# The first matmul of each MLP layer by Strassen's seven block products

## The chip, the cores and the metric

The kernel runs on one core of a Trainium2 chip. The metric is the device time of one execution in microseconds: 992.04 us is the median of 3 runs before the change (991.65 to 992.12).

## The reference

Causal attention with a decay over 4 x 8 heads of 576 tokens and width 64 is followed by two MLP layers over all 2304 tokens. Everything is float32.

```
scores = q @ k.T / 8 + decay, causal;  attn = softmax(scores) @ v      # (2304, 512) over all heads
h = x @ w_in            # 512 -> 2048
g = relu(h) ** 2        # layer 1
x = g @ w_out           # 2048 -> 512
h = x @ w_in            # layer 2
g = h where h >= 1, 0 where h <= -1, else (h + 1) ** 2 / 4
out = g @ w_out
```

## The kernel before

Each float32 operand of a matmul is split into a high part (rounded to the type fp32r) and a low part (the rest), and each product is three matmuls: high x high, high x low, low x high. The high part is a copy on ScalarE, the low part a subtraction on VectorE (on GpSimd for q, k, v and the first weights).

The attention goes over 16 pairs of heads as a software pipeline. The order of the work on each engine is written out by hand in lists (PE_ORDER, ACT_ORDER, DVE_ORDER, and PE_LAST, ACT_LAST, DVE_LAST for the last step, in which the first pieces of layer 1 stand among the last ones of the attention). The letters are pieces of work: T transposes of probabilities and their splits, O products with v, R the reciprocals of the sums, M the writing of x, U the first matmul of a tile, W a weight split, G a g tile.

The MLP layers then take the tokens in five chunks of 384, 512, 512, 512 and 384. In a chunk, j runs over the 16 tiles of 128 columns of the hidden width. `up(layer, c, j)` (L1140 to L1168) computes h of tile j from 4 slices of the model width, 12 matmuls, into one of four PSUM banks. ScalarE and VectorE turn h into g, high and low (`relu2`, L702 and L908, in layer 1; `smooth2`, L712 and L915, in layer 2). `down1` (L1172) and `down2` (L1189) add tile j's part of the second matmul into four other banks, 12 matmuls in a chunk of 512; in layer 1 g streams and w_out is stationary, in layer 2 it is the other way round. TensorE runs up of tile j ahead of down of tile j - 2.

All weights of a layer lie in SBUF, high and low (W). They are loaded once a layer through the sync queue (`load_w`, L434) and split once. GpSimd splits the first four weight tiles and the first x chunk during the last attention steps and then has nothing more to do. At the end of a chunk ScalarE and VectorE copy y from PSUM to x (`put_y1`, `put_y2`); the last chunk is stored tile by tile (L498 to L504).

All engines are in order and wait for each other by counting semaphores.

## Time and profile before

| | us |
|---|---|
| median of 3 runs | 992.04 |
| profiled execution | 991.63 |
| its span on the core | 989.80 |
| TensorE (PE) busy | 983.0 |
| VectorE (DVE) busy | 516.8 |
| ScalarE (ACT) busy | 405.3 |
| GpSimd (POOL) busy | 153.0 |

The profiler records each instruction of one execution. The page has busy times and the clock over 40 slices of the span; other views are tables by stretch of time, groups of instructions by source line and shape, the chain of waits, and the instructions in order of time. Times of single instructions are us from the span's start. Matmuls are pipelined: their own durations overlap, so their pace is read from the starts of successive groups.

### The profile page before, as it was taken

The numbers are of one execution on the slowest core, as the hardware profiler recorded it, in microseconds if no ns is written. First come the engines' busy times: TensorE is split into PE (matmuls) and PEld (weight loads), VectorE is DVE, ScalarE is ACT, GpSimd is POOL, SyncE is SP. The second block draws the span as 40 slices with busy tenths as digits, with TensorE's granted clock in tenths as the row PEclk, the third lists the DMA queues.
The fourth block names the chain that finished last, engine by engine and source line by source line (L and its number), as shares of the span: only waits on it lengthen the run. The fifth ranks groups of instructions, "written<-read, shape, count | busy, mean of one in ns | idle before, by whom it ended". The sixth has DMA issues, their size and how long they took to land.

```text
span 989.8 us, 14986 instructions
## 1 busy us (share of the span) xinstructions
PE 983.0 (99%) x5266; PEld 859.0 (87%) x5266; DVE 516.8 (52%) x1079; ACT 405.3 (41%) x888; POOL 153.0 (15%) x208
## 2 busy tenths in 40 slices
PE   8999999999999999999999999999999999999998
PEld 7888888999988888888889998988888888888997
DVE  7888888765422332232233566555455445544544
ACT  7888888854322232232223454232222223223322
POOL 7877888600000000000000000000000000000000
PEclk9999999999999999999999999999999999999999
DMA  6445555232000000000002440000001000000100
GB/s 220 147 145 177 158 175 195 65 121 72 1 1 1 1 0 0 0 0 1 1 1 64 127 129 22 1 32 1 1 1 43 0 0 33 10 1 1 43 1 32
DMA packets 39473, 50.01 MB, mean 51 GB/s; under 512 B 2656, under 2 KB 26720, under 8 KB 39424
## 3 DMA queue, kind: packets, MB, share of 16 engines
q1 hardware_dynamic: 39424, 49.37, 15.6%
q8 instruction: 30, 0.49, 0.2%
q14 instruction: 19, 0.16, 0.1%
HBM read 44.56 MB, written 4.79 MB: 50 GB/s over the span
## 4 chain that ended last, share of the span: by engine, by line
PE 96%; DVE 2%; ACT 1%; issue 0%; DMA 0%
PE banks L1167 39%; PE banks L1198 19%; PE banks L1184 19%; PE banks L1121 7%; PE banks L1066 5%; PE banks L1076 5%; PE banks L1092 1%; PE banks L1125 1%; PE banks L1117 0%; ACT W L689 0%; DMA fs<-f_dram 0%; DVE W L894 0%; DVE r L928 0%; DVE r L922 0%; ACT r L716 0%
## 5 line engine op out<-in xcount | busy, mean ns | idle before, releaser
L1167 PE MATMUL banks<-xs,W 128*128 128x512 f32 (+1 forms) x1728 | 383.7, 371 | 0.0
L1167 PEld LDWEIGHTS banks<-xs,W 128*128 128x128 f32 x1728 | 317.9, 188 | 47.4
L1198 PE MATMUL banks<-W,gs 128*128 128x512 f32 x864 | 209.1, 390 | 0.2 <-DVE gs L905 0.2
L1184 PE MATMUL banks<-gs,W 128*128 128x512 f32 (+1 forms) x960 | 209.0, 367 | 0.0
L1184 PEld LDWEIGHTS banks<-gs,W 128*128 128x128 f32 x960 | 175.1, 188 | 22.5
L1198 PEld LDWEIGHTS banks<-W,gs 128*128 128x128 f32 x864 | 161.7, 188 | 32.9 <-DVE gs L905 0.5
L905 DVE TENSOR_TENSOR gs<-r,gs 128x512 fp32r<-128x512 f32 (+1 forms) x160 | 102.3, 639 | 113.0 <-ACT gs L710 62.1
L716 ACT ACTIVATE r<-r 128x512 f32<-128x512 f32 (+1 forms) x80 | 47.2, 590 | 217.2 <-DVE r L924 217.2
L912 DVE TENSOR_TENSOR r<-r 128x512 f32<-128x512 f32 (+1 forms) x80 | 51.0, 638 | 160.9 <-ACT r L707 160.9
L707 ACT ACTIVATE r<-banks 128x512 f32<-128x512 f32 (+1 forms) x80 | 44.3, 554 | 177.3 <-PE banks L1167 176.5
L922 DVE TENSOR_SCALAR r<-banks 128x512 f32<-128x512 f32 (+1 forms) x80 | 50.9, 636 | 76.0 <-PE banks L1167 75.7
L1121 PE MATMUL banks<-pT,vs 128*128 128x448 f32 (+2 forms) x384 | 86.9, 348 | 0.0
L660 ACT ACTIVATE pr<-pr,nmax 128x576 f32<-128x576 f32 (+2 forms) x144 | 82.7, 581 | 0.6 <-DVE nmax L862 0.6
L928 DVE TENSOR_TENSOR r<-banks,r 128x512 f32<-128x512 f32 (+1 forms) x80 | 51.1, 639 | 50.2 <-ACT r L716 50.0
L710 ACT ACTIVATE gs<-r 128x512 fp32r<-128x512 f32 (+1 forms) x80 | 47.2, 590 | 70.3 <-DVE r L912 53.8
L847 DVE TENSOR_TENSOR pT<-banks,pT 128x256 fp32r<-128x256 f32 (+1 forms) x144 | 70.0, 515 | 7.7 <-ACT pT L666 5.9
L666 ACT ACTIVATE pT<-banks 128x256 fp32r<-128x256 f32 (+1 forms) x144 | 61.5, 459 | 25.7 <-PE banks L1076 24.0
L719 ACT ACTIVATE gs<-r 128x512 fp32r<-128x512 f32 (+1 forms) x80 | 47.2, 589 | 57.0 <-DVE r L928 55.3
L1076 PE MATMUL banks<-ident,pr 128*128 128x128 f32 x384 | 60.9, 274 | 0.2 <-ACT pr L660 0.2
L1121 PEld LDWEIGHTS banks<-pT,vs 128*128 128x128 f32 x384 | 57.6, 190 | 0.9
L1066 PE MATMUL banks<-qk 128*128 128x288 f32 (+4 forms) x480 | 56.9, 328 | 0.0
L1066 PEld LDWEIGHTS banks<-qk 64*128 64x128 f32 (+1 forms) x480 | 42.8, 186 | 10.6 <-issue 6.8
(87 smaller groups left out, 692.7 us busy)
## 6 DMA issues: line engine op xcount, KB each, us to landing
qk_raw<-qk_dram SPq DMA_DIRECT2D x15, 608.0 KB, 6.2
W_raw<-moe_w_in_dram SPq DMA_DIRECT2D x32, 256.0 KB, 2.8
W_raw<-moe_w_out_dram SPq DMA_DIRECT2D x32, 256.0 KB, 3.0
cb<-cum_scratch SPq DMA_DIRECT2D x30, 256.0 KB, 4.4
v_raw<-v_dram SPq DMA_DIRECT2D x16, 320.0 KB, 5.3
cbt<-cum_scratch SPq DMA_DIRECT2D x30, 144.0 KB, 3.0
out_dram<-x SPq DMA_DIRECT2D x3, 1024.0 KB, 4.2
out_dram<-x SPq DMA_DIRECT2D x1, 768.0 KB, 3.5
```

The lines of the kernel that those rows point to most:

```text
L660: nc.scalar.activation(t, t, ACT.Exp, bias=nmax[:, par, u:u + 1], scale=-1.0, accum_out=rsum[:, par, u:u + 1]).then_inc(exp_done, 1)
L666: last = nc.scalar.activation(in_pT(part, 0), in_bank(part, n, par), copy)
L847: last = V.tensor_tensor(in_pT(part, 1), in_bank(part, n, par), in_pT(part, 0).bitcast(F32), ALU.subtract)
L905: V.tensor_tensor(gs[:, j % GR, 1, 0:width(c)], r[:, j % RR, 0:width(c)], gs[:, j % GR, 0, 0:width(c)].bitcast(F32), ALU.subtract).then_in ...
L912: V.tensor_tensor(t, t, t, ALU.mult).then_inc(g_done, 1)
L928: V.tensor_tensor(t, h_ps(j, c), t, ALU.max).then_inc(g_done, 1)
L1066: last = mm(score_ps(u, WIDTH[u])[:, n0:n1], qk2[rows, par, a, i * P:(i + 1) * P], qk2[rows, par, b, QW + n0:QW + n1], start=(t == 0 and n ...
L1076: last = turn(ps[:, c:c + P], pr[:, par, OFF[u] + j * P:OFF[u] + (j + 1) * P], ident[:, :])
L1121: last = mm(out_ps[:, c:S - P], vj, pT[:, b, u + (2 if j == 0 else 0):u + LEN[j], :].rearrange("p u c -> p (u c)"), start=False, stop=(n = ...
L1167: last = mm(h_ps(j, c, layer == 0), W[:, j, a, 0, t * P:(t + 1) * P], xs_of(layer, c)[:, b, t, 0:width(c)], start=(t == 0 and a == b), sto ...
L1184: last = mm(banks[:, t, 0:width(c)], W[:, j, a, 1, t * P:(t + 1) * P], gs[:, j % GR, b, 0:width(c)], start=(j == 0 and a == b == 0), stop= ...
L1198: last = mm(banks[:, t, :], gs[:, j % GR, a, t * P:(t + 1) * P], W[:, j, b, 1, :], start=(j == 0 and a == b == 0), stop=(j == FT - 1 and a ...
```

## The change

The 2304 tokens are taken in three chunks of 768, and the hidden tiles in eight pairs ("groups") a chunk, 48 groups over both layers, numbered q. For a group the first matmul is a product of 2 x 2 blocks: w_in of the pair (model width in two halves, tile pair in two) with x (model width in two halves, tokens in two halves of 384). Seven block products stand in for eight; each is 6 matmuls of 384 columns. Their weight operands are blocks of w_in or sums of them, their x operands blocks of x or sums of them.

- The raw w_in and w_out of a group are loaded anew for every chunk (`load_wi`, two transfers of 256 KB, and `load_wo`, one of 512 KB). GpSimd forms the five sums of w_in (`sum_w`), ScalarE and VectorE split the seven operands in two pieces (`split_wi`, of 1024 and 768 columns), and ScalarE and GpSimd split w_out (`split_wo`). For the next chunk GpSimd forms five sums of x (`sum_x`), and ScalarE and VectorE split seven x operands of 768 columns (`split_x`).
- Products go to two PSUM banks in turn; 5 and 6 are accumulated onto 3 and 4. ScalarE copies products 0, 1 and 3 to SBUF (`copy_product`), VectorE combines them with the others into the four h tiles of 384 columns (`combine`, c0 to c5; c0 has both inputs in SBUF, the others one in PSUM).
- g of a tile: ScalarE `gate`, VectorE `square`, ScalarE `hi_g`, VectorE `lo_g`. In layer 2, gate is relu(h / 2 + 1 / 2) and square is two instructions, a scalar_tensor_tensor and a tensor_tensor max.
- TensorE runs the products of group q with the blocks of the second matmul of group q - 1 among them (`unit`): 8 units in layer 1, each 3 matmuls of 512 and 3 of 256 columns, 12 in layer 2, each 3 of 512. y takes six banks.

The diff at its core (the placing of the tiles in SBUF, the semaphores' names and the helpers for slices of x are left out):

```diff
-    CHS = [3 * P, 4 * P, 4 * P, 4 * P, 3 * P]
+    HALF = 3 * P
+    CW = 2 * HALF
+    CHUNKS = N // CW
+    GROUPS_W = FT // 2
+    TOTAL = 2 * CHUNKS * GROUPS_W
+    PRODUCTS_W = 7
+    W_CUT = [slice(0, 4), slice(4, 7)]
+    ADDS = 6
+    TILE_JJ = [1, 0, 1, 0]
+    TILE_HALF = [0, 1, 1, 0]
...
+    def units_of(q):
+        last = q % GROUPS_W == GROUPS_W - 1
+        if layer_of(q) == 0:
+            units = [(jj, d) for jj in (1, 0) for d in range(KT)]
+            if last:
+                units = [(jj, d) for d in range(KT) for jj in (1, 0)]
+        else:
+            units = [(TILE_JJ[k], 3 * TILE_HALF[k] + t) for k in range(4) for t in range(3)]
+            if last:
+                units = [(jj, t) for t in range(TILES_Y) for jj in (1, 0)]
+        return units
+    def per_slot(q):
+        if q % GROUPS_W == GROUPS_W - 1:
+            return [2, 2, 2, 2, 0, 0, 0] if layer_of(q) == 0 else [3, 3, 3, 3, 0, 0, 0]
+        return [1, 1, 1, 1, 1, 1, 2] if layer_of(q) == 0 else [2, 2, 2, 2, 2, 1, 1]
...
     SyncE
+            def load_wi(n):
+                if n >= SLOTS:
+                    sp.wait_ge(p_done, PRODUCTS_W * (n - SLOTS + 1))
...
+            def load_wo(n):
+                if n >= SLOTS:
+                    sp.wait_ge(y_done, units_before(n - SLOTS + 1))
...
...
     GpSimd
+            def sum_w(n):
+                slot = n % SLOTS
+                pool.wait_ge(wi_in[slot], 32 * (n // SLOTS + 1))
+                for to, a, b, op in W_SUMS:
+                    last = nc.gpsimd.tensor_tensor(wi_raw[slot][:, to, :], wi_raw[slot][:, a, :],
+                                                   wi_raw[slot][:, b, :], op)
+                last.then_inc(w_summed, 1)
...
+            for q in range(1, TOTAL):
+                split_wo(q)
+                if q + 2 < TOTAL:
+                    sum_w(q + 2)
+                g = q % GROUPS_W
+                if 2 <= g < 7 and chunk_of(q) + 1 < 2 * CHUNKS:
+                    sum_x(chunk_of(q) + 1, g - 2)
...
     ScalarE
+            def group(q):
+                c, g = chunk_of(q), q % GROUPS_W
+                old = c - 1 if g == 0 else None
+                new = c + 1 if g == GROUPS_W - 1 and c + 1 < 2 * CHUNKS else None
+                gate(q - 1, 3)
+                copy_product(q, 0)
+                hi_g(q - 1, 3)
+                if old is not None:
+                    split_x(c, 6)
+                if q + 1 < TOTAL:
+                    split_wi(q + 1, 0)
+                if new is not None:
+                    split_x(new, 0)
+                copy_product(q, 1)
+                if old is not None:
+                    put_y(old, 0)
+                if q + 1 < TOTAL:
+                    split_wi(q + 1, 1)
+                split_wo(q)
+                if new is not None:
+                    split_x(new, 1)
+                gate(q, 0)
+                if old is not None:
+                    put_y(old, 1)
+                hi_g(q, 0)
+                copy_product(q, 2)
...
+                gate(q, 1)
...
+                hi_g(q, 1)
...
+                gate(q, 2)
+                hi_g(q, 2)
...
...
     VectorE
+            COMBINE = [("e", 0, None, ALU.subtract), ("e", 1, 2, ALU.add), ("h", 0, 2, ALU.add),
+                       ("h", 1, 4, ALU.add), ("h", 2, 5, ALU.add), ("h", 3, 6, ALU.subtract)]
+            OTHER = [("s", 0), ("s", 0), ("s", 1), ("s", 2), ("e", 0), ("e", 1)]
...
+            def square(q, k):
+                dve.wait_ge(relued, 4 * q + k + 1)
+                h = h_tiles[k][:, :]
+                if layer_of(q) == 0:
+                    V.tensor_tensor(h, h, h, ALU.mult).then_inc(g_done, 1)
+                else:
+                    u = u_tiles[k % 2][:, :]
+                    V.scalar_tensor_tensor(u, u, 1.0, u, ALU.min, ALU.mult).then_inc(squared, 1)
+                    dve.wait_ge(squared, 4 * (q - CHUNKS * GROUPS_W) + k + 1)
+                    V.tensor_tensor(h, h, u, ALU.max).then_inc(g_done, 1)
...
+            def group(q):
+                square(q - 1, 3)
+                lo_g(q - 1, 3)
+                if old is not None and old >= 0:
+                    split_x(c, 5)
+                combine(q, 0)
+                if old is not None:
+                    split_x(c, 6)
+                    put_y(old, 0)
+                if new is not None:
+                    split_x(new, 0)
+                combine(q, 1)
+                combine(q, 2)
+                if q + 1 < TOTAL:
+                    split_wi(q + 1, 0)
+                square(q, 0)
...
+                lo_g(q, 0)
+                if q + 1 < TOTAL:
+                    split_wi(q + 1, 1)
+                combine(q, 3)
+                square(q, 1)
...
+                lo_g(q, 1)
+                combine(q, 4)
...
+                square(q, 2)
+                lo_g(q, 2)
+                combine(q, 5)
...
...
     TensorE
+            def product(q, i):
+                if i == 0:
+                    pe.wait_ge(wi_ready, 2 * q)
+                if q % GROUPS_W == 0:
+                    pe.wait_ge(xs_ready, PRODUCTS_W * chunk_of(q) + i + 1)
...
+                elif i == 0:
+                    pe.wait_ge(combined, ADDS * (q - 1) + 5)
+                elif i == 1:
+                    pe.wait_ge(combined, ADDS * q)
+                elif i == 2:
+                    pe.wait_ge(copied, 3 * q + 1)
+                elif i == 3:
+                    pe.wait_ge(copied, 3 * q + 2)
+                elif i == 4:
+                    pe.wait_ge(combined, ADDS * q + 3)
+                if i == 5:
+                    pe.wait_ge(copied, 3 * q + 3)
+                if i == 6:
+                    pe.wait_ge(combined, ADDS * q + 4)
+                for t in range(2):
+                    for a, b in TERMS:
+                        last = mm(ps, w[a][:, W_OF[i], t * P:(t + 1) * P], xs[i][:, b, t, :],
+                                  start=(i < 5 and t == a == b == 0), stop=(i not in (3, 4) and t == a == 1),
+                                  skip_group_check=True)
+                last.then_inc(p_done, 1)
...
+            def group(q):
+                n = 0
+                for i in range(PRODUCTS_W):
+                    product(q, i)
+                    for _ in range(per_slot(q - 1)[i]):
+                        unit(q - 1, n)
+                        n += 1
```

Unit 0 of a group waits for w_out's split (`split_wo` on GpSimd) and for the g tiles that it reads: in layer 1 the first four units for tiles 0 to 2 and the others for tile 3, in layer 2 three units a tile; in the last group of a chunk of layer 2 the first six units read tiles 0 and 3 in turn, the other six tiles 2 and 1. The very first unit waits for c5 of group 0. In the last attention step X stands for split_x, P for a product, C for copy_product, A for combine, H for split_wi, G for gate or square, K for hi_g or lo_g.

## Rows read from the trace of the kernel before

**Rows 1.** The page: busy us by engine, and the granted clock in 40 slices.
```profile
PE 983.0 (99%) x5266; PEld 859.0 (87%) x5266; DVE 516.8 (52%) x1079; ACT 405.3 (41%) x888; POOL 153.0 (15%) x208
...
PEclk9999999999999999999999999999999999999999
```

**Rows 2.** Table by stretch: length, busy PE, PEld, DVE, ACT, POOL, clock, DMA share, GB/s.
```profile
253.00:526.00 273.00, 273.00 (x1222) 228.10 (x1221) 81.07 (x122) 72.06 (x122) 0.00 (x0) 1.00 0.00 1
...
656.00:920.00 264.00, 264.00 (x1169) 218.97 (x1168) 132.30 (x212) 69.72 (x112) 0.00 (x0) 1.00 0.03 11
```

**Rows 3.** Chain of waits: start, us, engine, line, count (384 columns, then 512).
```profile
620.96 2.10 PE banks L1167 x12
...
669.42 2.72 PE banks L1167 x12
```

**Rows 4.** Instructions in order of time, TensorE: start, us, engine, line, operation.
```profile
188.46 0.52 PE L1125 MATMUL banks<-pT,vs 128*128 128x256 f32 x3
188.81 0.60 PE L1076 MATMUL banks<-ident,pr 128*128 128x128 f32 x4
```

**Rows 5.** Groups by line and shape, VectorE, two SBUF inputs: busy us, mean ns.
```profile
L912 DVE TENSOR_TENSOR r<-r 128x384 f32<-128x384 f32 x32 | 17.8, 556 | 18.9 <-ACT r L707 18.9
```

**Rows 6.** In order of time: a 384-column g tile of layer 2, VectorE and ScalarE.
```profile
601.03 1.22 DVE L894 TENSOR_TENSOR W<-W_raw,W 128x1024 fp32r<-128x1024 f32 x1 [0.39 <-ACT W L689]
...
602.17 0.55 DVE L922 TENSOR_SCALAR r<-banks 128x384 f32<-128x384 f32 x1
602.75 0.36 DVE L924 TENSOR_SCALAR r<-r 128x384 f32<-128x384 f32 x1
603.15 0.53 ACT L716 ACTIVATE r<-r 128x384 f32<-128x384 f32 x1 [2.15 <-DVE r L924]
...
603.71 0.56 DVE L928 TENSOR_TENSOR r<-banks,r 128x384 f32<-128x384 f32 x1 [0.59 <-ACT r L716]
604.30 0.53 ACT L719 ACTIVATE gs<-r 128x384 fp32r<-128x384 f32 x1 [0.62 <-DVE r L928]
604.73 1.05 ACT L689 ACTIVATE W<-W_raw 128x1024 fp32r<-128x1024 f32 x1
604.86 0.56 DVE L905 TENSOR_TENSOR gs<-r,gs 128x384 fp32r<-128x384 f32 x1 [0.59 <-ACT gs L719]
```

**Rows 7.** Groups by line and shape, GpSimd, two inputs.
```profile
L527 POOL TENSOR_TENSOR qk<-qk_raw,qk 128x1216 fp32r<-128x1216 f32 x15 | 42.1, 2807 | 1.2
...
L541 POOL TENSOR_TENSOR vs<-v_raw,vs 128x320 fp32r<-128x320 f32 x32 | 27.2, 871 | 2.4 <-POOL vs L537 1.6
...
L619 POOL TENSOR_TENSOR W<-W_raw,W 128x512 fp32r<-128x512 f32 x8 | 10.3, 1291 | 0.7
```

**Rows 8.** In order of time, GpSimd and VectorE, and line 872's min/median/max ns.
```profile
110.30 2.81 POOL L527 TENSOR_TENSOR qk<-qk_raw,qk 128x1216 fp32r<-128x1216 f32 x1
...
112.29 0.56 DVE L847 TENSOR_TENSOR pT<-banks,pT 128x384 fp32r<-128x384 f32 x1
112.77 0.37 DVE L872 TENSOR_SCALAR rsum<-rsum 128x9 f32<-128x9 f32 x1
...
L872 DVE TENSOR_SCALAR rsum<-rsum x16: 161/184/1255, 20.0 to 195.2; 128x9 f32<-128x9 f32 x16
```

**Rows 9.** In order of time near the start, and the mean of line 537.
```profile
6.38 1.22 POOL L593 TENSOR_SCALAR cum<-cum 32x576 f32<-32x576 f32 x1 [0.72 <-DVE cum L832]
...
7.04 1.17 DVE L841 TENSOR_TENSOR cum_part<-cum,cum_part 128x576 fp32r<-128x576 f32 x1
...
7.68 1.70 POOL L537 TENSOR_SCALAR vs<-v_raw 128x320 fp32r<-128x320 f32 x2
...
L537 POOL TENSOR_SCALAR vs<-v_raw 128x320 fp32r<-128x320 f32 x32 | 14.9, 484 | 0.1
```

**Rows 10.** In order of time: the attention's last writes, and the last copy.
```profile
208.17 0.59 DVE L887 TENSOR_TENSOR x<-banks,rbc 64x128 f32<-64x128 f32 x2
...
986.61 0.60 ACT L814 ACTIVATE x<-banks 128x512 f32<-128x512 f32 x1 [0.76 <-PE banks L1198]
```

More of the change, by code:

```diff
@@ L300, in last_x, with x_part @@
[L300 to L309 removed]
+        def x_part(c, kt, half):
+            t = x[:, c * CW * KT:(c + 1) * CW * KT].rearrange("p (s b k n) -> p s k b n", s=2, k=KT, n=XB)
+            return t[:, half, kt]
@@ L311, in mixed_attention_mlp @@
+        ENDS = [(t, 0, D) for t in range(TILES_Y)]
         gates = sem("gates")
@@ new lines, in sum_x @@
+            def sum_x(c, s):
+                if c == 0:
+                    pool.wait_ge(x_put, 9)
+                elif c < CHUNKS:
+                    pool.wait_ge(x_put, PAIRS + 1)
+                else:
+                    pool.wait_ge(y_put_s, 3 * (c - CHUNKS) + 3)
+                    pool.wait_ge(y_put_v, 3 * (c - CHUNKS) + 3)
+                need(pool, xs_ready, PRODUCTS_W * c)
+                (ka, ha), (kb, hb), op = X_SUMS[s]
+                for k in range(2):
+                    last = nc.gpsimd.tensor_tensor(by_block(xt[:, s, k, :]), x_part(c % CHUNKS, ka + k, ha),
+                                                   x_part(c % CHUNKS, kb + k, hb), op)
+                last.then_inc(xt_ready, 1)
@@ L817, in _ @@
+            for q in range(1, TOTAL):
+                group(q)
+            gate(TOTAL - 1, 3)
+            hi_g(TOTAL - 1, 3)
+            for k in range(0, len(ENDS), 2):
+                t, n0, n1 = ENDS[k]
+                act.wait_ge(last_done, k + 1)
+                nc.scalar.activation(y_tile(CHUNKS - 1, t)[:, n0:n1], banks[:, t, n0:n1], copy)\
+                    .then_inc(last_put[k], 1)
         @block.vector
@@ L954, in do @@
                     put_x(g, n, m, dt)
-                if what == "W":
-                    split_w(n)
+                if what == "X":
+                    split_x(0, n)
+                if what == "A":
+                    combine(0, n)
+                if what == "H":
+                    split_wi(1, n)
                 if what == "G":
-                    relu2(0, n)
+                    square(0, n)
+                if what == "K":
+                    lo_g(0, n)
             steps(dve, DVE_ORDER, DVE_LAST, do)
-            def chunk1(c, first=False, last=False):
-                if not first:
-                    split_x(0, c)
-                    relu2(c - 1, FT - 1)
-                    relu2(c, 0)
-                    put_y1(c - 1)
-                for j in range(AHEAD if first else 1, FT - 1):
-                    relu2(c, j)
-                    if first and j + 2 < FT:
-                        split_w(j + 2)
-                    if last and j >= AHEAD:
-                        split_w(FT + j - AHEAD)
@@ L1014, in _ @@
+            for q in range(1, TOTAL):
+                group(q)
+            square(TOTAL - 1, 3)
+            lo_g(TOTAL - 1, 3)
+            for k in range(1, len(ENDS), 2):
+                t, n0, n1 = ENDS[k]
+                dve.wait_ge(last_done, k + 1)
+                V.tensor_copy(y_tile(CHUNKS - 1, t)[:, n0:n1], banks[:, t, n0:n1]).then_inc(last_put[k], 1)
         @block.tensor
@@ L1205, in chunk @@
-            def chunk(layer, c, down, end=False):
-                up(layer, c, 1)
-                for j in range(2, FT):
-                    up(layer, c, j)
-                    down(c, j - 2)
-                down(c, FT - 2)
-                if end:
-                    down(c, FT - 1, last_done)
-                    return
-                up(layer, c + 1, 0) if not (isinstance(c, int) and c == CHUNKS - 1) else up(layer + 1, 0, 0)
-                down(c, FT - 1)
+                w = [wo_hi_t[q % SLOTS], wo_lo_t[q % SLOTS]]
```

752 lines of the change are left out of this document (389 added, 363 removed), and 13 rows, old and new, of tables (ACT_LAST, DVE_LAST, PE_LAST).

## The prediction

> **What bounds the kernel now.** I read the page first. Its busy line gives TensorE 983.0 of 989.8 us, and the clock line grants full speed in every slice [rows 1]. The table by stage then shows what the others do while TensorE is full: in layer 1 VectorE is busy 81 of 273 us, in layer 2 132 of 264, GpSimd 0 in both [rows 2]. The chain of waits runs through TensorE in equal pieces: twelve 384-column matmuls take 2.10 us, twelve 512-column ones 2.72 [rows 3], so 0.175 and 0.227 us each, start to start. Three 256-column ones take 0.35 us from their first to what follows [rows 4], 0.117 each. So both layers are bound by streamed columns, and only fewer columns can save.
>
> **The matmuls.** The first matmul of a layer has 960 instructions now, 576 of 512 columns and 384 of 384: 576 x 0.227 + 384 x 0.175 = 198 us. After it there are 3 chunks x 8 pairs of tiles ("groups") x 7 products x 6 = 1008 of 384 columns: 176 us. Saved 22 us a layer, 44 in all. The second matmul of layer 1 goes from the same 198 us to 576 x (0.227 + 0.117) = 198 us. That of layer 2 stays 864 x 0.227. If TensorE never waited, the time would be the profiled execution's 991.6 less 44, some 948. A group is 15.5 us of TensorE (7 x 1.05 for products and 8.2 for the second matmul), 48 groups in all.
>
> **What VectorE, ScalarE and GpSimd have to do in those 15.5 us.** All streams are strictly in order. Per group VectorE gets six combinations of 384 columns (c0 to c5), two halves of the new split of w_in (1024 and 768), and for each of four g tiles a square and a low part. In layer 2 the square is two instructions, a new scalar_tensor_tensor and a max. An operation of 384 columns with two SBUF inputs is 0.56 us [rows 5]; 1024 are 1.22 [rows 6], 768 by width 0.96. I price the scalar_tensor_tensor, which before doesn't have, at 0.56. Below it lies the one-input 0.36 [rows 6]; above it, an instruction that takes as long as one of twice the columns, 0.96.
>
> The order decides, not the busy time. "combine, square, lo_g" of tiles 1 to 3 stand directly behind one another, and each needs the one before it by way of ScalarE. From the 384-column tile in [rows 6]: VectorE ends, 0.03 later ScalarE starts, 0.53, 0.03 later VectorE starts. A relay is 0.59; an instruction that depends on its forerunner on VectorE starts 0.03 after its end; an independent one 0.08 before it. One tile of layer 2: combine 0.56, relay (gate) 0.59, two instructions 1.15, relay (hi_g) 0.59, low part 0.56, less 0.08: 3.37. Three are 10.1. The rest of the group: c0 to c2 at 0.48 each, first half of the split 1.14, square of tile 0 1.15, relay 0.59, low part 0.48, second half 0.88: 5.7. c0 also waits for ScalarE's copy of product 1, which stands behind half a split of w_in there (1.05), so it comes 0.87 later than VectorE is free. Sum 16.6 us, over TensorE's 15.5. In layer 1 a tile is 2.78 and the sum 14.3, under it.
>
> **GpSimd.** It idles in the layers today; after, every group has five additions of 256 columns (sum_w), one subtraction of 1024 (split_wo), and in five groups of eight two additions of 384 (sum_x). From 320, 512 and 1216 columns at 0.87, 1.29 and 2.81 [rows 7], a column costs 2.15 ns: 0.74, 2.40 and 1.01 us, or 6.1 to 8.1 a group. That fits in 15.5, and its data are early. But it isn't free to VectorE. In [rows 8] a nine-column VectorE operation on SBUF alone starts at 112.77 while GpSimd runs 110.30 to 113.11, and ends at 113.14: it took 0.37, in the worst of the 16 cases 1.25, against 0.16 at best. The VectorE operation just ahead of it, one input in PSUM, took its usual 0.56 beside the same GpSimd instruction. [Rows 9] show it for two SBUF inputs and for both orders: L841 (576 columns, 0.76 by width) starts at 7.04 under GpSimd's 6.38 to 7.60 and ends 0.61 after that; GpSimd's next two, which queue behind L841, together take 1.70 where one is 0.48 on average. So an operation of VectorE with both inputs in SBUF and one of GpSimd exclude each other, and where both queue they alternate, each counting its length less 0.15. The combinations c1 to c5 read PSUM and are free of this; c0, squares, low parts and splits are not.
>
> The Trainium skill has this as a rule ("SBUF — State Buffer", section "Who interferes with whom"): a VectorE instruction with two SBUF inputs contends with a GpSimd instruction that reads SBUF, and the one that comes second blocks fully. The trace agrees in those rows; by the rule the sum is the one below, without it the second rival's.
>
> Laid on the order: ScalarE ends split_wo's high part 3.0 us after hi_g of the last group's tile 3; GpSimd's 2.40 then starts when VectorE's first split half ends at 4.0, ends at 6.25, and the square of tile 0 waits for it: +2.2. Its five additions come behind one by one. One goes between the two instructions of the square (+0.4), two into the relay (+0.4), one ahead of the second half (+0.5), one under c3 (0). So c3 starts at 10.5 where it would at 7.0, and a group of layer 2 takes **20.1 us**; with sum_x, which falls on tile 1, 21.0. In layer 1 the same gives 17.3, or 18.2 if product 2 comes a little late and GpSimd gets in before the split; I take **17.8**. TensorE isn't the limit then: its first product waits for c4 of the group before, 14.4 us into a cycle of 20.1.
>
> Ends of chunks: five x splits (0.96, partly in relays) and ScalarE's ahead of the copy, +2.9 a last group (+2.6 in layer 1); in the first group y must be whole early, so product 1 stands behind two blocks of the second matmul that need tile 3, and two x splits and a put_y follow: +3.7 (+3.5).
>
> **The turn from attention to layer 1.** The attention's last result lands at 208.8 [rows 10], with four first-matmul tiles (8.4 us) in TensorE's gaps; the seven products (7.3) take their place. VectorE gets seven x splits and four combinations before it for two g tiles and a weight split, some 4 us more, of which its idle time takes most: 210. From there split w (2.0), tiles 0 to 2 and c4, c5 end near 220, and TensorE's first block waits for that c5. With tile 3's square and the third sum_w in between, hi_g of tile 3 is at 222.
>
> **Sum.** 222; 23 cycles of layer 1 at 17.8, 409, plus two first and three last groups, 15; 24 of layer 2 at 20.1, 482, plus ten with sum_x, 9, three first and two last, 17; the end: low part 0.6, eleven blocks of three matmuls 7.5, and copy and store as now, 989.8 less 986.6 [rows 10], 3.2. Total 1165, and 1.8 that the execution lies over its span: **1167 us**. The profiled execution is 0.4 under the median of 992.04, which changes nothing here. DMAs: 1 MB a group, 68 GB/s, with slots freed a whole group ahead; I charge none, and a late one would cost what it is late.
>
> **Rivals.**
> 1. scalar_tensor_tensor at the upper bound, 0.96: +0.4 x 4 x 24 = 38 us, 1205. Nothing before speaks to it. The Trainium skill does ("Vector Engine (DVE) Microarchitecture Reference", "Points that are easy to get wrong"): such an instruction with two SBUF sources that aren't bf16 halves its throughput; no row here shows one. 13%.
> 2. GpSimd hinders little (its work falls in VectorE's waits): layer 1 bound by TensorE, layer 2 by 16.6. 222 + 23 x 15.5 + 24 x 16.6 + some 20 at chunks + 13 = 1010. For it: half of VectorE's cycle is relay; against it [rows 8, 9]. 9%.
> 3. Faster: the relays don't add up, because c3 to c5 find their products early and VectorE catches up at each chunk. Then TensorE's columns decide: 948, with the turn 958. It needs a layer-2 group of 15.5; it would be level at about 16.3 (992 less 958, less some 15 at chunks, over 24). Against it is the written order, which has nothing between combine and square. 4%.
> 4. TensorE's clock falls. It has 15.5 us of work in 20.1, its longest wait about 2 us; the attention stage, with gaps too, was granted full speed throughout [rows 1]. At 1.2 GHz a group would be 31 us, and layer 2 alone cost 250 more: 1400. 3%.
>
> **Numbers.** The forecast has 71%; its own range is 1095 to 1200, since each of the 47 cycles can be off by a microsecond where GpSimd's turn falls otherwise. For eight in ten I take 1055 to 1225, which takes in the first rival and half the way to the second. This kernel's measurements tell about 0.2% from no change: faster 4%, same 1%, slower 95%.
>
> **What would show it.** Right: in layer 2 the chain of waits runs through VectorE and ScalarE; TensorE waits before product 0 for a VectorE combination; squares, low parts and splits have means well over 0.56 (0.8 and more for tile 0's), the combinations that read PSUM keep 0.56; GpSimd's busy time is over 400 us. A layer-2 group of 16 to 17 us with means of 0.56 makes rival 2; a scalar_tensor_tensor of 0.96, rival 1. The forecast is wrong if TensorE is over 95% busy in layer 2, or if VectorE operations with two SBUF inputs keep 0.56 beside GpSimd.

## The result: 23% slower

The kernel after takes **1222.79 us** (four runs, 1220.77 to 1225.53), the kernel before 991.85 (four runs, 991.64 to 992.12): a ratio of 1.233, with a 95% interval of 1.230 to 1.236. Forecast were 1167, with 1055 to 1225. The profiled execution took 1221.12 us, with a span of 1219.3.

The page of the kernel after: busy us by engine, the granted clock in 40 slices, and the summary by engine and line of the chain that ended last. It answers to [rows 1].

```profile
PE 1027.1 (84%) x5554; PEld 884.7 (73%) x5554; DVE 894.5 (73%) x1443; ACT 594.6 (49%) x1217; POOL 598.9 (49%) x536
...
PEclk9999999799999999999999899899899999899998
...
DVE 40%; PE 38%; ACT 13%; issue 8%; DVEq 0%; ACTq 0%; POOL 0%; POOLq 0%
```

TensorE is idle 192 us where it was idle 7, GpSimd works 599 us where it worked 153, and only 38% of the chain lies on TensorE. The table by stretch (columns as in [rows 2]), one stretch of each layer (layer 1's groups end near 682):

```profile
470.00:700.00 230.00, 197.69 (x1044) 173.73 (x1043) 164.75 (x203) 102.73 (x178) 114.27 (x86) 0.97 0.18 53
700.00:950.00 250.00, 198.50 (x877) 166.04 (x875) 185.94 (x239) 100.54 (x170) 107.37 (x80) 0.94 0.18 55
```

TensorE is busy 86% of layer 1's stretch and 79% of layer 2's, where [rows 2] had it full, and VectorE isn't full either (72 and 74%): the time is in waits between engines. They aren't waits for transfers: GpSimd waited for weights only twice, both times at the turn (10.4 and 22.6 us, the second for weights that are split a group later). The groups by line and shape of VectorE and ScalarE (busy us, mean ns of one, idle before it) show who pays:

```profile
L1131 DVE TENSOR_TENSOR gs<-h_tile,gs 128x384 fp32r<-128x384 f32 x192 | 133.5, 696 | 101.6 <-ACT gs L896 101.6
L1083 DVE TENSOR_TENSOR wi_lo<-wi_raw,wi_hi 128x1024 fp32r<-128x1024 f32 x47 | 104.3, 2219 | 0.0
L1125 DVE SCALAR_TENSOR_TENSOR u_tile<-u_tile 128x384 f32<-128x384 f32 x96 | 97.3, 1014 | 47.1 <-ACT u_tile L888 47.1
L1122 DVE TENSOR_TENSOR h_tile<-h_tile 128x384 f32<-128x384 f32 x96 | 71.8, 747 | 38.4 <-ACT h_tile L884 38.4
L1127 DVE TENSOR_TENSOR h_tile<-h_tile,u_tile 128x384 f32<-128x384 f32 x96 | 69.7, 726 | 3.3
L1083 DVE TENSOR_TENSOR wi_lo<-wi_raw,wi_hi 128x768 fp32r<-128x768 f32 x47 | 68.4, 1455 | 0.0
L1114 DVE TENSOR_TENSOR h_tile<-e_tile,banks 128x384 f32<-128x384 f32 x96 | 52.4, 546 | 0.0
...
L1114 DVE TENSOR_TENSOR e_tile<-s_tile,s_tile 128x384 f32<-128x384 f32 x48 | 26.8, 558 | 62.4 <-ACT s_tile L877 62.4
...
L888 ACT ACTIVATE u_tile<-h_tile,half 128x384 f32<-128x384 f32 x96 | 59.2, 617 | 118.8 <-DVE h_tile L1114 117.9
L884 ACT ACTIVATE h_tile<-h_tile 128x384 f32<-128x384 f32 x96 | 50.4, 525 | 125.0 <-DVE h_tile L1114 124.7
```

The low parts, splits of w_in and squares, all with two SBUF inputs, have means well over what [rows 5, 6] have for their widths; the combinations that read PSUM keep 0.54 to 0.55. One with two SBUF inputs isn't raised: c0 (e_tile from s_tile and s_tile) keeps 0.56. In the group of layer 1 shown under e10 it runs at 468.51, when GpSimd has been idle for 6.8 us and starts again only at 470.14.

Below, all cycles are counted from one start of hi_g of tile 3 (the fourth L896 of a group) to the next. With them the forecast's sum stands beside the trace:

```
term                              forecast   measured
hi_g of tile 3 of group 0            222       234.5     +12.5
23 cycles of layer 1                 424       447.5     +23.5   (middle 17.8: 18.9)
24 cycles of layer 2                 508       522.4     +14.4   (middle 20.1 / 21.0 with sum_x: 20.6 / 21.6)
end                                   11.3      14.9      +3.6
```

**One group of layer 2** (VectorE, ScalarE and GpSimd in order of time: start, us), from the middle of a chunk:

```profile
775.65 1.22 DVE L1083 TENSOR_TENSOR wi_lo<-wi_raw,wi_hi 128x1024 fp32r<-128x1024 f32 x1
775.73 3.39 POOL L746 TENSOR_TENSOR wo_lo<-wo_raw,wo_hi 128x1024 fp32r<-128x1024 f32 x1 [10.95 <-ACT wo_hi L869]
...
776.79 2.75 DVE L1125 SCALAR_TENSOR_TENSOR u_tile<-u_tile 128x384 f32<-128x384 f32 x1
779.08 5.17 POOL L718 TENSOR_TENSOR wi_raw<-wi_raw 128x256 f32<-128x256 f32 x5
779.57 0.98 DVE L1127 TENSOR_TENSOR h_tile<-h_tile,u_tile 128x384 f32<-128x384 f32 x1
...
781.15 1.10 DVE L1131 TENSOR_TENSOR gs<-h_tile,gs 128x384 fp32r<-128x384 f32 x1 [0.59 <-ACT gs L896]
782.17 1.49 DVE L1083 TENSOR_TENSOR wi_lo<-wi_raw,wi_hi 128x768 fp32r<-128x768 f32 x1
...
784.21 2.29 POOL L761 TENSOR_TENSOR xt<-x 128x384 f32<-128x384 f32 x2
784.81 0.82 DVE L1125 SCALAR_TENSOR_TENSOR u_tile<-u_tile 128x384 f32<-128x384 f32 x1 [0.68 <-ACT u_tile L888]
785.67 1.25 DVE L1127 TENSOR_TENSOR h_tile<-h_tile,u_tile 128x384 f32<-128x384 f32 x1
```

A cycle of 21.6 can be added up from these rows. The square of tile 0 waits until GpSimd's subtraction is over and ends 0.42 us after it (779.12 to 779.54): 2.19 over its free 0.56. Then 0.42 on the max, 0.54 on the low part and 0.54 on the second half of the split, each for one of the five additions, and 0.26 and 0.69 on tile 1 for the two x sums: 4.64. With the forecast's 16.6 of order and four gates at 0.62 instead of 0.53 (0.36) that is 21.6.

### The profile page after: what moved, and what is told of

It is laid out like the page before. It is cut to its first block, busy times and chain, and to the rows that moved or that the text cites. A ratio compares the mean times of both kernels' runs of the same rounds, so it can differ in the third digit from the quotient of the medians.

```text
span 1219.3 us, 16869 instructions
## 1 busy us (share of the span) xinstructions
PE 1027.1 (84%) x5554; PEld 884.7 (73%) x5554; DVE 894.5 (73%) x1443; ACT 594.6 (49%) x1217; POOL 598.9 (49%) x536
## 4 chain that ended last, share of the span: by engine, by line
DVE 40%; PE 38%; ACT 13%; issue 8%; DVEq 0%; ACTq 0%; POOL 0%; POOLq 0%
PE banks L1384 10%; DVE wi_lo L1083 10%; DVE u_tile L1125 7%; DVE h_tile L1114 6%; PE banks L1422 6%; ACT gs L896 5%; DVE h_tile L1127 5%; PE banks L1329 5%; PE banks L1430 4%; PE banks L1274 4%; DVE h_tile L1122 4%; DVE gs L1131 4%; PE banks L1284 3%; PE banks L1424 3%; ACT u_tile L888 3%
## 5 line engine op out<-in xcount | busy, mean ns | idle before, releaser
L1384 PE MATMUL banks<-xs,wi_hi 128*128 128x384 f32 x1344 | 367.7, 355 | 136.1 <-DVE h_tile L1114 83.1
L746 POOL TENSOR_TENSOR wo_lo<-wo_raw,wo_hi 128x1024 fp32r<-128x1024 f32 x48 | 131.5, 2739 | 528.8 <-ACT wo_hi L869 528.7
L1384 PEld LDWEIGHTS banks<-xs,wi_hi 128*128 128x128 f32 x1344 | 238.0, 194 | 201.2 <-issue 72.3
L718 POOL TENSOR_TENSOR wi_raw<-wi_raw 128x256 f32<-128x256 f32 x240 | 263.4, 1130 | 32.9 <-DMA wi_raw<-moe_w_in_dram 32.9
L896 ACT ACTIVATE gs<-h_tile 128x384 fp32r<-128x384 f32 x192 | 100.6, 524 | 307.9 <-DVE h_tile L1127 180.2
L1384 PE MATMUL banks<-xs,wi_lo 128*128 128x384 f32 x672 | 231.2, 344 | 0.0
L1430 PE MATMUL banks<-wo_hi,gs 128*128 128x512 f32 x576 | 216.5, 413 | 14.0 <-DVE gs L1131 14.0
L1131 DVE TENSOR_TENSOR gs<-h_tile,gs 128x384 fp32r<-128x384 f32 x192 | 133.5, 696 | 101.6 <-ACT gs L896 101.6
L1422 PE MATMUL banks<-gs,wo_hi 128*128 128x512 f32 x384 | 147.4, 405 | 33.0 <-DVE gs L1131 31.1
L1083 DVE TENSOR_TENSOR wi_lo<-wi_raw,wi_hi 128x1024 fp32r<-128x1024 f32 x94 | 172.6, 1837 | 0.0
L1125 DVE SCALAR_TENSOR_TENSOR u_tile<-u_tile 128x384 f32<-128x384 f32 x96 | 97.3, 1014 | 47.1 <-ACT u_tile L888 47.1
L1384 PEld LDWEIGHTS banks<-xs,wi_lo 128*128 128x128 f32 x672 | 130.4, 194 | 0.0
L888 ACT ACTIVATE u_tile<-h_tile,half 128x384 f32<-128x384 f32 x96 | 59.2, 617 | 118.8 <-DVE h_tile L1114 117.9
L884 ACT ACTIVATE h_tile<-h_tile 128x384 f32<-128x384 f32 x96 | 50.4, 525 | 125.0 <-DVE h_tile L1114 124.7
L1122 DVE TENSOR_TENSOR h_tile<-h_tile 128x384 f32<-128x384 f32 x96 | 71.8, 747 | 38.4 <-ACT h_tile L884 38.4
```

What stands on the lines that cost most here:

```text
L718: last = nc.gpsimd.tensor_tensor(wi_raw[slot][:, to, :], wi_raw[slot][:, a, :], wi_raw[slot][:, b, :], op)
L746: nc.gpsimd.tensor_tensor(wo_lo_t[slot][:, :, :].rearrange("p a n -> p (a n)"), raw, hi.bitcast(F32), ALU.subtract).then_inc(wo_ready, 1)
L896: nc.scalar.activation(g_part(q, k, 0), h_tiles[k][:, :], copy).then_inc(g_hi, 1)
L1083: V.tensor_tensor(wi_lo_t[slot][:, part, :].rearrange("p a n -> p (a n)"), wi_raw[slot][:, 1 + part.start:1 + part.stop, :].rearrange("p a ...
L1122: V.tensor_tensor(h, h, h, ALU.mult).then_inc(g_done, 1)
L1125: V.scalar_tensor_tensor(u, u, 1.0, u, ALU.min, ALU.mult).then_inc(squared, 1)
```

## The experiments

The theory is the forecast's: VectorE's order with its relays through ScalarE sets a cycle of 16.6 (layer 2) or 14.3 us (layer 1), and GpSimd's exclusion adds the rest. The rivals are that one of the two alone explains it, that TensorE's work is the bound, or that the waits lie elsewhere. Each kernel ran once with a profile, beside the kernel before (991.4 to 992.7 us on the same chips). Middle cycles (the usual length of a cycle in the middle of a chunk) and total:

```
kernel             us      layer 1   layer 2 (with / without sum_x)   clock
after              1221.1   18.9      21.6 / 20.6                      0.963
e1_no_pool         1061.2   15.6      16.9                             0.974
e2_pipelined       1102.9   17.1      18.2 / 17.4                      0.975
e3_both            1016.2   15.6      15.7                             0.981
e4_two_terms       1196.2   17.8      21.5 / 20.6                      0.916
e5_no_sum_w        1151.8   17.7      19.9 / 19.1                      0.974
e10_split_first    1203.4   18.2      20.9 / 20.1                      0.958
e7_pipe2           1064.3   15.7      17.0 / 15.7                      0.968
e8_bound           1027.6   15.7      17.0 / 15.7                      0.985
e9_turn            1018.9   15.7      17.0 / 15.7                      0.990
e11_turn_no_pool    980.8   15.6      15.7                             0.993
```

**GpSimd's work left out.** In the layers GpSimd only counts. The sums of w_in are replaced from the fourth group on by transfers of plain blocks, the sums of x from the second chunk on by x itself (not shown below), and w_out's low part from group 1 on by its high part; so a part of the computation is missing.

```diff
-                pool.wait_ge(wi_in[slot], 32 * (n // SLOTS + 1))
+                pool.wait_ge(wi_in[slot], 32 + 80 * (n // SLOTS))
+                if n > 2:
+                    pool.sem_inc(w_summed, 1)
+                    return
                 for to, a, b, op in W_SUMS:
...
+                if n > 0:
+                    pool.sem_inc(wo_ready, 1)
+                    return
                 nc.gpsimd.tensor_tensor(wo_lo_t[slot][:, :, :].rearrange("p a n -> p (a n)"), raw, hi.bitcast(F32),
```

> GpSimd does nothing in the layers: the sums of w_in are replaced by three more transfers of plain w_in blocks from group 3 on (0.6 MB a group more), the sums of x by x itself from chunk 1 on, and w_out's high part stands in for its low part. VectorE, ScalarE and TensorE do the same instructions. Theory (VectorE operations with two SBUF inputs and GpSimd's exclude each other): the weight split of 1024 columns falls from a mean of 2.2 to 1.22 us, low parts from 0.70 to 0.56, a group of layer 1 from 18.9 to 15.6 (TensorE's own), one of layer 2 from 21.6 to 17.0 (the chain of relays, with ScalarE's gate at its measured 0.62): 1219 - 23 x 3.3 - 24 x 4.6 = about 1035. Rival (the relays alone make the cycle, and GpSimd's work would be hidden): within 15 us of 1221. Rival (weight transfers are late or slow VectorE): more transfers, so over 1221.

160 us go. The groups by line of VectorE in this kernel, the same operations of the same shapes:

```profile
L1148 DVE TENSOR_TENSOR gs<-h_tile,gs 128x384 fp32r<-128x384 f32 x192 | 108.2, 564 | 101.8 <-ACT gs L913 101.8
L1100 DVE TENSOR_TENSOR wi_lo<-wi_raw,wi_hi 128x1024 fp32r<-128x1024 f32 x47 | 57.3, 1219 | 0.0
L1139 DVE TENSOR_TENSOR h_tile<-h_tile 128x384 f32<-128x384 f32 x96 | 53.9, 561 | 38.4 <-ACT h_tile L901 38.4
L1144 DVE TENSOR_TENSOR h_tile<-h_tile,u_tile 128x384 f32<-128x384 f32 x96 | 53.6, 558 | 3.3
L1142 DVE SCALAR_TENSOR_TENSOR u_tile<-u_tile 128x384 f32<-128x384 f32 x96 | 53.4, 556 | 47.2 <-ACT u_tile L905 47.2
```

The split half falls from 2219 to 1219 ns, scalar_tensor_tensor from 1014 to 556, and the idle time before each line stays (47.2 and 47.1, 38.4 and 38.4): in these lines the exclusion sits in the durations and the relays in the idle time. The cycles come to 15.6 and 16.9, against 15.6 and 17.0 expected. The total is 26 us more than expected, at the turn (237.9) and in the groups around a change of chunk (23 to 25 us for the first of layer 2).

**VectorE's order alone.** Each low part stands behind the next combination, and the second half of the split fills tile 0's relay.

```diff
                     split_x(new, 1)
-                lo_g(q, 0)
                 if q + 1 < TOTAL:
...
                 combine(q, 3)
+                lo_g(q, 0)
                 square(q, 1)
```

> Only VectorE's order is changed: lo_g of tile k comes after the combination of tile k+1, and the second half of the w_in split ahead of c3, so that each relay through ScalarE has another VectorE instruction beside it. Nothing is left out. Theory: the written order (combine, square, lo_g back to back) costs three relays a group; layer 2 falls from 21.6 to about 18.3 us a group, layer 1 from 18.9 to about 16.5, sum about 1085. Rival (only the exclusion with GpSimd matters, the waits are filled by it anyway): no more than 20 us off 1221, since VectorE and GpSimd still have to take turns.

118 us go with GpSimd's work untouched: the idle time before the low parts falls from 101.6 us to 44.2. Expected were 136; layer 1's cycle came to 17.1 instead of 16.5. With both edits in one kernel:

> The order of e2_pipelined and no GpSimd work in the layers as in e1_no_pool (the same parts of the computation are left out). Theory: both causes gone, TensorE is the limit in both layers at 15.5 us a group: 234 for all before, 23 x 15.6 + 24 x 15.5, some 30 at the ends of chunks, 15 at the end: about 1010. If either cause is not one, this equals e1_no_pool or e2_pipelined.

Alone they save 160 and 118, together 205, less than the 278 of the sum, because in both layers the cycle now is TensorE's own, 15.6 to 15.7. So neither cause is "the" cause: relays and exclusion lie on one chain, and each is worth what the other leaves over TensorE's floor.

**Less work for TensorE.** The second matmul leaves out its third term, a third of its 8.2 us a group.

```diff
-                        for a, b in TERMS:
+                        for a, b in TERMS[0:2]:
```

> The second matmul of both layers leaves out its third term (high x low of one side): 96 instead of 144 matmul pieces, 2.7 us of TensorE less in each of 48 groups, nothing else. Theory (VectorE's chain sets the cycle): under 25 us off 1221, from the ends of chunks and the last group. Rival (TensorE's columns, or its clock, set the cycle): 100 to 130 us off.

The third terms are 130 us of columns at the full clock (48 times 2.7). TensorE's busy time falls by 87, since the granted clock falls to 0.916 as well, and the total by 25. Layer 2's middle cycles don't move (21.5). Most of the 25 us come from layer 1's, which fall from 18.9 to 17.8 though TensorE isn't their bound; expected was a gain at the ends of chunks and in the last group. In order of time, the start of a group there:

```profile
481.87 1.22 DVE L1083 TENSOR_TENSOR wi_lo<-wi_raw,wi_hi 128x1024 fp32r<-128x1024 f32 x1
...
482.10 3.23 POOL L746 TENSOR_TENSOR wo_lo<-wo_raw,wo_hi 128x1024 fp32r<-128x1024 f32 x1 [7.16 <-ACT wo_hi L869]
```

VectorE's split half comes before GpSimd's subtraction and takes its free 1.22. In the kernel after it is the other way round in layer 1, as the rows under e10 below show, because VectorE waits 0.44 us for a product first.

**The five additions of GpSimd alone.** Only the first part of e1's edit; the subtraction on w_out and the x sums stay.

```diff
+                if n > 2:
+                    pool.sem_inc(w_summed, 1)
+                    return
                 for to, a, b, op in W_SUMS:
```

> Of GpSimd's work only the five additions of w_in are taken away (replaced by transfers of plain w_in blocks from group 3 on, which leaves the sums out); the subtraction of 1024 columns for w_out and the sums of x stay, and the order is that of the changed kernel. The full price of GpSimd's work is 3.3 us a group in layer 1 (18.9 to 15.6) and 4.7 in layer 2 (21.6 to 16.9), as e1_no_pool showed. Theory (each GpSimd instruction blocks for its own length where it meets a VectorE one): the long one alone costs about 2.2 us and the x sums about 0.9, so a group without the additions takes about 17.5 in layer 1 and 19.7 in layer 2, sum about 1145. Rival (the number of GpSimd instructions counts, not their length): nearly all goes with the additions, about 1075.

69 us for the additions; the other 91 of e1's 160 belong to one subtraction of 1024 columns a group and two x sums in five groups of eight. In layer 2 the cycle falls by 1.7 us, where the rows of the group above charge the additions with 0.42 + 0.54 + 0.54.

**The subtraction held back behind the split half.** The forecast laid its order so.

```diff
             for q in range(1, TOTAL):
+                if q + 1 < TOTAL:
+                    pool.wait_ge(wi_ready, 2 * q + 1)
                 split_wo(q)
```

> The changed kernel with one more wait: GpSimd starts its subtraction on w_out only when VectorE has done the first half of its weight split. The forecast laid its order on this assumption and got 17.3 us for a group of layer 1 (17.8 taken) and 20.1 for one of layer 2; measured were 18.9 and 20.6 to 21.6 with the subtraction ahead of the split half. If that order was the cause of layer 1's miss: a group in the middle of layer 1 takes 17.3 to 17.8 instead of 18.9, the split half falls from 2.2 to about 1.3 us on average, and the time falls by 20 to 30 us. Rival, the order costs nothing since GpSimd's 2.4 us are paid either way (they then fall on the square of tile 0): cycles stay within 0.3 us of 18.9 and the time within 10 us of 1222.

The time falls by 18 us, just short of the 20 to 30 expected, and layer 1's cycle is 18.2, not 17.3 to 17.8. Both layers gain in the middle of a chunk: 18.9 becomes 18.2, 21.6 and 20.6 become 20.9 and 20.1. But only 5 of the 18 us come from layer 1, where two groups of the first chunk take 19.7 and the second groups of the later chunks rise from 18.4 and 19.3 to 20.2; 14 come from layer 2. In order of time, layer 1 in the kernel after:

```profile
469.52 0.55 DVE L1114 TENSOR_TENSOR e_tile<-s_tile,banks 128x384 f32<-128x384 f32 x1 [0.44 <-PE banks L1384]
469.99 0.55 DVE L1114 TENSOR_TENSOR h_tile<-s_tile,banks 128x384 f32<-128x384 f32 x1
470.14 2.41 POOL L746 TENSOR_TENSOR wo_lo<-wo_raw,wo_hi 128x1024 fp32r<-128x1024 f32 x1 [8.43 <-ACT wo_hi L869]
470.45 3.18 DVE L1083 TENSOR_TENSOR wi_lo<-wi_raw,wi_hi 128x1024 fp32r<-128x1024 f32 x1
```

and in e10:

```profile
472.38 1.22 DVE L1085 TENSOR_TENSOR wi_lo<-wi_raw,wi_hi 128x1024 fp32r<-128x1024 f32 x1
...
473.52 0.55 DVE L1124 TENSOR_TENSOR h_tile<-h_tile 128x384 f32<-128x384 f32 x1
473.68 2.64 POOL L746 TENSOR_TENSOR wo_lo<-wo_raw,wo_hi 128x1024 fp32r<-128x1024 f32 x1 [8.43 <-DVE wi_lo L1085]
...
474.66 2.08 DVE L1133 TENSOR_TENSOR gs<-h_tile,gs 128x384 fp32r<-128x384 f32 x1 [0.59 <-ACT gs L898]
```

After the wait of 0.44 for TensorE's product, the subtraction is 0.31 us ahead of the split half and costs it 1.96. Held back, it lets the split and the square of tile 0 through and costs the low part 1.52. So who comes first by a third of a microsecond moves a cycle by half a microsecond or more, but the 2.4 us are paid somewhere.

**Better orders, with the whole computation.** e7 takes e2's order further: ScalarE's copies and VectorE's splits are laid into the remaining relays, on both engines (ScalarE's list is shown).

```diff
                 gate(q - 1, 3)
+                if q + 1 < TOTAL:
+                    split_wi(q + 1, 0)
                 copy_product(q, 0)
                 hi_g(q - 1, 3)
...
-                if q + 1 < TOTAL:
-                    split_wi(q + 1, 0)
+                copy_product(q, 1)
```

> Nothing is left out. On top of e2_pipelined the last unfilled relays are filled: the first half of the w_in split stands between square and lo_g of tile 3, its second half between c2 and the square of tile 0, and ScalarE copies product 1 right behind hi_g of tile 3. Theory: VectorE then has hardly any relay left to wait for (e2: 17.1 and 18.2 us a group); what stays is its own 10 to 12 us and some 4 of GpSimd's, so layer 1 comes to TensorE's 15.6 to 16 and layer 2 to about 16.3, sum about 1025. Rival (in e2_pipelined the exclusion alone was left, its total of locked time being the limit): under 15 us off e2_pipelined's 1103.

The middle of the chunks does as intended, 15.7, and 17.0 where x sums fall; the mean of the first split half is 1218 ns, so nothing stands in its way any more. The total is 39 us over what was expected: the two groups around a change of chunk take 42 us in layer 1 (19.0 and 22.9) and 44 in layer 2. e8 changes these alone: it orders the last group's blocks so that none needs tile 3 early (not shown), spreads them over its products, and copies first the banks that are done first:

```diff
-            return [2, 2, 2, 2, 0, 0, 0] if layer_of(q) == 0 else [3, 3, 3, 3, 0, 0, 0]
+            return [2, 2, 1, 1, 1, 1, 0] if layer_of(q) == 0 else [3, 3, 2, 2, 1, 1, 0]
...
-    Y_ACT = [[0, 4, 2], [0, 2, 4]]
-    Y_DVE = [[1, 3, 5], [1, 3, 5]]
+    Y_ACT = [[0, 4, 5], [3, 5, 1]]
+    Y_DVE = [[1, 2, 3], [4, 0, 2]]
```

> e7_pipe2, and at the ends of chunks the blocks of the second matmul stand in an order in which none needs tile 3 early, and are spread over six product slots instead of four; banks are copied out in the order in which they become whole. Nothing is left out. Theory: the waits of 1 to 4.4 us of TensorE at five chunk ends and in the last group (22 us in sum in e3_both) go to some 8: 10 to 15 us less than e7_pipe2. Rival (they are due to the x splits): under 4 us.

37 us, three times what was expected: the first group of a chunk falls from 22.9 to 16.9 in layer 1 and from 23.6 and 24.8 to 17.6 in layer 2, and the end is 3 us shorter, since the last blocks no longer begin with one that needs the last low part. e9 changes only the order of the turn's lists, so that the x splits come earlier on VectorE and ScalarE and the low parts of the first g tiles later (VectorE's list as its letters, X an x split, A a combination, H a high or low part of w, K a low part of g):

```diff
-X2 T5 A0 X3 T6 X4 A1 A2 X5 A3 M0 X6 M1 H0 H1 G0 K0 G1 K1 A4 G2 K2 A5
+X2 T5 X3 T6 X4 A0 A1 A2 X5 H0 M0 X6 M1 H1 A3 G0 K0 G1 A4 K1 G2 A5 K2
```

> e8_bound, and in the last attention step ScalarE splits x operands 3, 5 and 6 ahead of work that waits for later matmuls, VectorE takes c0 behind x operands 3 and 4 and the g tiles interleaved. Nothing is left out. Theory: hi_g of tile 3 of group 0 came at 234.6 us instead of the 222 of the forecast since single waits of in-order engines were linked in a ring (TensorE 3.7 and 4.3 us for x splits, VectorE 7.6, ScalarE 6.9); now it comes 8 to 14 us earlier. Rival (the turn is bound by the sum of work there): under 3 us.

hi_g of tile 3 of group 0 comes at 229.6 instead of 237.4, and the total is 9 us less. This is the best kernel with all of the computation, 1018.9 against 991.4: 2.8% slower than before.

**The same order without GpSimd's work**: e1's edit on e9.

> The order of e9_turn without the additions and subtractions of GpSimd in the layers (left out: the weight sums from the fourth group on, the x sums and w_out's low part, as in e1_no_pool). If what keeps e9_turn above the kernel before is GpSimd's hindrance to VectorE at the chunk ends (19 to 20 us a last group) and beside the x sums (17.0 against 15.7 us in layer 2), all groups come to 15.7, the last ones too, and the time is 975 to 985 us, under the 991.4 of before. Rival, the ends of chunks are bound by the x splits themselves, which must follow the last group's products: last and first groups of a chunk stay 3 us or more over 15.7 together, and the time is 990 to 1005.

The page's busy line, and the turn and most of layer 1 in the table by stretch:

```profile
PE 955.2 (98%) x5554; PEld 866.2 (88%) x5554; DVE 722.1 (74%) x1443; ACT 591.2 (60%) x1217; POOL 163.9 (17%) x214
```

```profile
189.00:240.00 51.00, 36.66 (x190) 33.24 (x191) 33.24 (x58) 26.44 (x58) 12.96 (x12) 0.87 0.23 65
240.00:600.00 360.00, 359.27 (x2071) 335.75 (x2070) 238.23 (x395) 200.00 (x348) 0.00 (x0) 1.00 0.39 110
```

980.8 against 992.7, inside the 975 to 985 expected. GpSimd's hindrance is worth the last 38 us, and TensorE then loses next to nothing in the layers (359.27 of 360 us busy). One point was missed: the last groups of a chunk in layer 2 take 18.4, not 15.7, and the two after them 15.8 and 14.0, with TensorE busy throughout (359.08 of 360 us from 600 to 960). Of the 44 us of columns saved, 12 arrive even so, in a kernel that leaves a part of the computation out. The table by stretch gives 14 us of idle TensorE at the turn (36.66 of 51.00 busy) and some 5 from its clock there (0.13 of 36.66); 8 more are 47 cycles of 15.76 on average instead of 15.6, which is the forecast's 176 and 198 us over 24 groups; the last 5 are not traced. Storing the split weights in the first chunk and loading them in the other two would take GpSimd out of 32 of 48 groups, save for the x sums. By an estimate from e9 and e11 that is at most two thirds of 38 us: 1018.9 less 25, level with before. It was not tried.

## Why the prediction was right

**The range held by luck.** 1222.79 lies 2.2 us under the upper end of 1055 to 1225, and one of the four runs (1225.53) lies above it; the narrower range, 1095 to 1200, was missed. The 54 us between the sum and the span all point the same way, in each of the four terms above. What was right is the mechanism.

**The mechanism and both its parts.** TensorE is 79% busy in layer 2, its products wait for VectorE's combinations, squares and splits are long where both inputs are in SBUF, the PSUM combinations keep 0.55, and GpSimd works 599 us. e1, e2 and e3 show order and exclusion apart. The rule on the two engines that the forecast quoted from the Trainium skill ("SBUF — State Buffer", section "Who interferes with whom") holds, also in that GpSimd waits: its subtraction, queued 0.08 us behind the split half, takes 3.39 where it takes 2.41 alone.

**Group of layer 2: forecast 20.1 and 21.0, measured 20.6 and 21.6.** The four prices of the exclusion were 2.2, 0.4, 0.4, 0.5; the rows have 2.19, 0.42, 0.54, 0.54, and 0.95 for sum_x where 0.9 was charged. The mis-sized term is the relay through the gate: 0.53 was taken from a plain activation [rows 6], and with a bias from a tile and a scale it took 617 ns (L888) against 525 (L884), 0.09 x 4. The rest is 0.2 of the additions.

**Group of layer 1: forecast 17.8, measured 18.9.** This is the largest miss, 23.5 us in all. The working named both orders, 17.3 with the split half first and 18.2 with GpSimd ahead if product 2 comes late, and took the middle. The trace has the second, with a wait of 0.44 for that product; in e4, where TensorE has less to do ahead of it, the wait and the order are gone and the cycle is 17.8. And it charged the x sums in layer 2 only; in layer 1 they cost 0.51 (squares of 0.93 and low parts of 0.70 on tile 1, against 0.56). 18.2 + 0.5 = 18.7. e10 moves the order and gets 18.2 and not 17.3; the x sums cost 1.3 us of it (0.09, 0.56 and 0.64 over).

**The turn: forecast 222, measured 234.5.** The step "VectorE has some 4 us more, of which its idle time takes most: 210" failed. The attention's last result came at 222.57, 14.4 us after [rows 10]. In order of time, TensorE with its waits and that last write:

```profile
206.98 0.61 PE L1384 MATMUL banks<-xs,wi_hi 128*128 128x384 f32 x2 [3.52 <-DVE xs L1078]
...
217.94 0.68 PE L1384 MATMUL banks<-xs,wi_hi 128*128 128x384 f32 x2 [4.09 <-DVE xs L1078]
...
222.57 0.59 DVE L1064 TENSOR_TENSOR x<-banks,rbc 64x128 f32<-64x128 f32 x2
```

A product stands in TensorE's list ahead of the attention's own blocks and waits for an x split, which stands in VectorE's list behind ScalarE's high part, which waits for TensorE. The forecast added VectorE's work and didn't walk the three lists against one another. e9, which only reorders them, gets 8 us back against e8 (229.6 for 237.4). TensorE's clock fell too, to 0.86 on average from 189 to 230. How the rest divides between waits and clock stays open.

**First groups of a chunk and the end.** Layer 2's first groups took 26.0 to 26.7, where 20.1 + 3.7 was the forecast; layer 1's took 21.8 and 23.2, for 17.8 + 3.5. TensorE in order of time in the first group of layer 2's second chunk, and its table by stretch (columns as in [rows 2]):

```profile
856.54 0.40 PE L1430 MATMUL banks<-wo_hi,gs 128*128 128x512 f32 x1
861.46 0.80 PE L1430 MATMUL banks<-wo_hi,gs 128*128 128x512 f32 x1 [4.52 <-DVE gs L1131]
...
862.47 1.06 PE L1430 MATMUL banks<-wo_hi,gs 128*128 128x512 f32 x2
```

```profile
861.00:866.00 5.00, 4.54 (x12) 3.99 (x13) 1.27 (x2) 1.49 (x2) 0.00 (x0) 0.50 0.01 3
866.00:870.00 4.00, 4.00 (x18) 3.50 (x18) 2.21 (x4) 2.66 (x4) 0.92 (x1) 0.89 0.01 2
870.00:874.00 4.00, 4.00 (x21) 3.43 (x20) 3.97 (x5) 1.10 (x2) 4.00 (x3) 1.00 0.00 0
```

A block of the second matmul stands in the list behind product 0 and needs the low part of tile 3, which comes 4.5 us later. And then TensorE runs at 1.2 GHz, with 0.43 us a matmul of 512 columns instead of 0.23, until about 867. The end shows the same: 4.94 us of waiting for the last low part, then 0.43 a matmul for 5.7 us.

```profile
1205.58 0.80 PE L1430 MATMUL banks<-wo_hi,gs 128*128 128x512 f32 x1 [4.94 <-DVE gs L1131]
```

```profile
1205.50:1208.00 2.50, 2.42 (x6) 1.94 (x7) 0.02 (x1) 0.60 (x1) 0.00 (x0) 0.50 0.03 7
```

Thirteen matmuls up to 1211.29 at 0.2 us more each are 2.6 of the end's 3.6 us. Layer 1's two first groups show the price side by side. In both, the same block waits 1.56 us for the low part of the same tile:

```profile
370.85 0.50 PE L1422 MATMUL banks<-gs,wo_hi 128*128 128x512 f32 x1 [1.56 <-DVE gs L1131]
...
525.90 0.80 PE L1422 MATMUL banks<-gs,wo_hi 128*128 128x512 f32 x1 [1.56 <-DVE gs L1131]
```

After the first the granted clock stays full, after the second it is 0.5 for 3 us. From then on the instructions of all engines come 1.4 us later in the second group than in the first, and it takes 23.2 us instead of 21.8.

The fourth rival, a clock that falls in every group, did not come: the granted clock of the two stretches above is 0.97 and 0.94. But in small it was in the sum, where the forecast had nothing for it.

**The first rival**, scalar_tensor_tensor at 0.96, is refuted. Its shortest and median durations in the kernel after:

```profile
L1125 DVE SCALAR_TENSOR_TENSOR u_tile<-u_tile x96: 549/559/2765, 693.6 to 1203.2; 128x384 f32<-128x384 f32 x96
```

With GpSimd's work left out the mean is 556 ns. In both kernels its two sources are the same tile. The rule quoted from the Trainium skill ("Vector Engine (DVE) Microarchitecture Reference", "Points that are easy to get wrong"), a halved throughput with two SBUF sources that aren't bf16, doesn't show at 384 fp32 columns: 0.56 is what a tensor_tensor of that shape takes. **The second rival**, GpSimd hinders little, asked for 1010; leaving its work out gives 1061, so 160 us hung on it. **The third**, faster, had TensorE's columns decide; even without GpSimd's work and with the better order the total is 981, not 958.

## What to carry to other kernels

Count what a saving on the busiest engine asks of the others in the order in which they do it: write one steady cycle down with its relays, then lay every GpSimd instruction against VectorE's operations with two SBUF inputs, one for one. That gave 20.1 and 21.0 for cycles of 20.6 and 21.6, where busy shares (73, 49 and 49%) would have promised room. Then walk the places that aren't steady as carefully, list against list; there 16 us of the turn and the end were missed, and reordering the ends of chunks and the turn alone was worth 45 us (e7 to e9). Before adding work to an idle GpSimd, ask which VectorE operations run beside it.

## What the runs showed of the hardware

- From 240 us on, TensorE's granted clock fell to 1.2 GHz sixteen times in the kernel after, for 3 to 6 us each. It did so at all three waits of 4.5 to 4.9 us (for some 5.5, 3 and 5.7 us after 861.46, 1041.13 and 1205.58), but also at a wait of 2.16 us (881.77, for 6 us). Of the waits of 2.46 us in the middle groups of layer 2, some had it (766.95) and some didn't (745.40 and 810.27), and those cycles differ by no more than 0.2 us. So the length of the last wait alone doesn't tell; the forecast, which had the longest at 2 us, priced none. The granted clock over the span was 0.963 in the kernel after, 0.990 in e9 and 0.916 in e4, which gives TensorE the least work in nearly the same cycles.
- An activation with a bias tile and a scale took 617 ns at 384 columns, a plain one 525, a copy from PSUM to SBUF 473.
- Where VectorE and GpSimd exclude each other, the duration that the profile shows contains the wait: a mean over the free duration (2219 against 1219 ns) is the sign to look for, since the idle columns show nothing (0.0 us before L1083).
